# A weight ring of six buffers, a hand-over between two splitting engines, and q and k loads that wait for the gates

## The reference

```python
for t in range(S):
    m_new = np.maximum(f_gate[:, :, t] + m, i_gate[:, :, t])
    f_stab = np.exp(f_gate[:, :, t] + m - m_new)
    i_stab = np.exp(i_gate[:, :, t] - m_new)
    C = f_stab * C + i_stab * np.einsum('bhd,bhe->bhde', vt, kt)
    n = f_stab * n + i_stab * kt
    h_tilde = np.einsum('bhde,bhe->bhd', C, qt)
    denom = np.maximum(np.abs(np.einsum('bhd,bhd->bh', n, qt)), 1.0)
    y[:, :, t] = sigmoid(o_gate[:, :, t]) * h_tilde / denom
```

```python
x = (sigmoid(x @ w_gate) * (x @ w_val)) @ w_out            # layer 1
xn = x / np.sqrt(np.mean(x * x, -1) + 1e-6) * rms_g
x = (silu(xn @ w2_gate) * (xn @ w2_val)) @ w2_out          # layer 2
```

## Time and profile before

| what | value |
|---|---|
| median of 3 runs | 450.21 us (450.01 to 450.27) |
| the profiled execution | 450.15 us |
| its span, first to last instruction | 447.9 us |
| TensorE (PE) busy | 443.5 us, 99% |
| VectorE busy | 217.7 us, 49% |
| ScalarE busy | 183.6 us, 41% |
| GpSimd busy | 87.4 us, 20% |
| DMA traffic | 26.69 MB |

### The profile page before, as it was taken

One profiled execution on the slowest core, in us unless ns is written; L12 is line 12 of the kernel. 1 busy time (PEld: TensorE's weight loads), 2 busy tenths in 40 slices (PEclk: granted clock), 3 DMA queues, 4 the chain that ended last, 5 costly groups with the idle time before them and its releaser, 6 DMA issues.

```text
span 447.9 us, 10560 instructions
## 1 busy us (share of the span) xinstructions
PE 443.5 (99%) x4491; PEld 405.7 (91%) x4491; DVE 217.7 (49%) x475; ACT 183.6 (41%) x358; POOL 87.4 (20%) x131
## 2 busy tenths in 40 slices
PE   8999999999999999999999999999999999999997
PEld 5899999999999999988889988889988899888897
DVE  6879827854565456414432227560055730256510
ACT  7886277544753473214543154331033320133310
POOL 3569610112010200004656181000000000000000
PEclk9999999999999999999999999999999999999999
DMA  8975500321122114000433010000000000000000
GB/s 240 299 262 167 140 3 3 82 82 35 51 80 69 37 31 143 19 1 14 148 106 113 22 44 1 1 0 31 31 2 0 1 16 29 16 2 1 0 31 29
DMA packets 10430, 26.69 MB, mean 60 GB/s; under 512 B 1504, under 2 KB 4608, under 8 KB 10384
## 3 DMA queue, kind: packets, MB, share of 16 engines
q1 hardware_dynamic: 10128, 25.96, 19.1%
q10 hardware_dynamic: 256, 0.07, 0.1%
HBM read 23.97 MB, written 1.97 MB: 58 GB/s over the span
## 4 chain that ended last, share of the span: by engine, by line
PE 98%; DMA 1%; SPq 0%; ACT 0%; issue 0%
PE bank L1205 37%; PE bank L1156 21%; PE bank L1224 10%; PE bank L1226 9%; PE bank L1225 9%; PE bank L1063 3%; PE bank L1094 3%; PE bank L997 2%; PE bank L1082 1%; PE bank L1033 1%; PE bank L1103 1%; DMA step<-in_qk_t 1%; PE bank L1236 0%; PE bank L1249 0%; PE bank L1257 0%; PE bank L1047 0%
## 5 line engine op out<-in xcount | busy, mean ns | idle before, releaser
L1205 PE MATMUL bank<-x_hi,wgv_hi 64*128 64x512 f32 x576 | 106.0, 388 | 0.0
L676 ACT ACTIVATE sg<-bank 128x256 f32<-128x256 f32 (+1 forms) x96 | 47.1, 491 | 131.7 <-PE bank L1205 82.7
L1205 PE MATMUL bank<-x_lo,wgv_hi 64*128 64x512 f32 x480 | 94.0, 387 | 0.0
L947 DVE TENSOR_TENSOR bank<-sg,bank 128x256 f32<-128x256 f32 (+1 forms) x96 | 53.7, 560 | 55.8 <-ACT sg L676 54.1
L1156 PE MATMUL bank<-x_hi,wgv_hi 128*128 128x256 f32 x288 | 80.5, 291 | 0.0
L1156 PE MATMUL bank<-x_lo,wgv_hi 128*128 128x256 f32 x288 | 77.8, 283 | 0.0
L1224 PE MATMUL bank<-wo_hi,h_hi 128*128 128x320 f32 x240 | 75.5, 314 | 0.0
L1205 PE MATMUL bank<-x_hi,wgv_lo 64*128 64x512 f32 x384 | 75.2, 387 | 0.0
L1226 PE MATMUL bank<-wo_hi,h_lo 128*128 128x320 f32 x240 | 74.2, 309 | 0.0
L1225 PE MATMUL bank<-wo_lo,h_hi 128*128 128x320 f32 x240 | 74.2, 309 | 0.0
L945 DVE TENSOR_TENSOR sg<-sg,bank 128x512 f32<-128x512 f32 x36 | 24.8, 688 | 83.0 <-ACT sg L676 83.0
(11 more groups left out here) (143 smaller groups left out, 540.4 us busy)
## 6 DMA issues: line engine op xcount, KB each, us to landing
step<-in_qk_t SPq DMA_DIRECT2D x24, 192.0 KB, 3.8
step<-in_vok SPq DMA_DIRECT2D x12, 324.0 KB, 3.0
step<-in_w_gv SPq DMA_DIRECT2D x6, 576.0 KB, 3.7
raw_p<-in_w_gv SPq DMA_DIRECT2D x4, 576.0 KB, 5.2
raw_x<-in_w_gv SPq DMA_DIRECT2D x4, 576.0 KB, 6.7
step<-in_vok SPq DMA_DIRECT2D x10, 160.0 KB, 4.4
raw_p<-in_w_o SPq DMA_DIRECT2D x3, 480.0 KB, 3.2
y<-y_tok SPq DMA_DIRECT2D x9, 160.0 KB, 1.8
```

Source lines behind the costliest of these rows:

```text
L676: act.activation(sg_view(n), g_view(n), ACT.Sigmoid).then_inc(sg_done, 1)
L947: dve.tensor_tensor(v_view(n), sg_view(n), v_view(n), ALU.mult).then_inc(hf_done, 1)
L1205: mm = pe.matmul(ps(n), w, x, start=own and (s, p) == (0, 0), stop=last and not own)
```

## The change

Four edits:

1. SP waits for the gates' semaphore before it issues the loads of q and k, and with them every later load.
2. There are six raw buffers. Chunks 0 and 1 get one each of their own, and chunks 2 to 11 go round a ring of the other four. Chunks 4 and 5 no longer wait for a split; the load of chunk 4 is issued ahead of q and k of tile 3.
3. ScalarE waits for the splits of chunks 0 and 1 at tile 2, and for the last split at tile 5 in place of tile 4, because the buffers lie under other tiles now.
4. GpSimd waits for VectorE's split of chunk 7 before it starts on chunk 6.

```diff
-            under("pad0", [P, 4 * CW])
-            raw_x0 = under("raw_x0", [P, 4 * CW])
+            under("pad0", [P, 2 * CW])
+            raw_x0 = under("raw_x0", [P, 3 * CW])
+            raw_x2 = under("raw_x2", [P, 3 * CW])
...
-            under("pad1", [P, 4 * CW])
-            raw_x1 = under("raw_x1", [P, 4 * CW])
+            under("pad1", [P, 2 * CW])
+            raw_x1 = under("raw_x1", [P, 3 * CW])
+            raw_x3 = under("raw_x3", [P, 3 * CW])
...
-        raw0 = [raw_p[:, :], raw_x0[:, 0:3 * CW], raw_x1[:, 0:3 * CW], raw_q[:, :]]
+        raw0 = [t[:, :] for t in (raw_p, raw_q, raw_x2, raw_x3, raw_x0, raw_x1)]
+        RING = len(raw0) - B
+
+        def raw0_at(c):
+            return RING + c if c < B else (c - B) % RING
...
             def load_raw0(c):
-                if c >= len(raw0):
-                    wait_split(sp, c - len(raw0))
+                if c >= B + RING:
+                    wait_split(sp, c - RING)
                 src, w = raw_src(0, c)
-                s = c % len(raw0)
+                s = raw0_at(c)
...
             sp.dma_start(fi_r[:, :, :], gates[:, :, :]).then_inc(gates_in, 16)
+
+            sp.wait_ge(gates_in, 16)
             load_qk(0)
             load_qk(1)
...
             load_qk(2)
             load_vo(2)
+            load_raw0(4)
             load_qk(3)
             load_kn(2)
-            load_raw0(4)
             load_raw0(5)
...
                         for c in SPLIT_AT.get(slot, []):
+                            if c == BY_VECTOR[-1] - 1:
+
+                                wait_split(pool, c + 1)
                             split(0, c)
...
-                    act.wait_ge(raw0_in[c % len(raw0)], 16 * (c // len(raw0) + 1))
+                    act.wait_ge(raw0_in[raw0_at(c)], 16 * (1 if c < B else (c - B) // RING + 1))
...
-                    if n == 4:
+                    if n == B:
+                        for c in range(B):
+                            wait_split(act, c)
+                    if n == 5:
                         wait_split(act, WCH - 1)
```

More of the change, by code:

```diff
@@ L217, in raw_of @@
         def raw_of(lay, c):
-            r = raw1[c % len(raw1)] if lay else raw0[c % len(raw0)]
+            r = raw1[c % len(raw1)] if lay else raw0[raw0_at(c)]
             if c < GVC:
```

## The result

| | median | lowest to highest | executions |
|---|---|---|---|
| before | 450.21 us | 449.88 to 450.27 | 5 |
| changed | 457.31 us | 455.58 to 458.79 | 5 |

The ratio is 1.0164, with a 95% interval of 1.0134 to 1.0194. I had forecast 451.9 and a range of 450.6 to 454.0: the direction was right, the size and the range were wrong.

The account below looks back on a forecast made before the run. TensorE's own list was taken as the bound, with q and k what its start waits for. Edit 1's +2.0 less 0.3 gave +1.7 us, the other edits 0; on 450.15 this made 451.9 us, range 450.6 to 454.0.

Parts of the forecast that it names:

- What bounds the kernel: Whole kernel: TensorE's list bounds it, 98% of the chain; at the start TensorE waits for q and k until 5.61.
- Edit 1, when the scores start: Kernel start: gates' signal at 3.4, q and k landing 4.15 us after issue, first scores at 7.64 against 5.65.
- the predicted +1.7: Edit 1's net term at the start: +2.0 us delay less 0.3 from faster scores, with ends +0.6 and +2.5.
- The port rule: Gates' load: 16 partitions make it slow by itself, so the signal stays near 3.64, the term near +2.0.
- The step that failed: First scores: at the higher clock they take 1.04 and not 1.30 us, giving 0.26 us back.
- The low clock: First block: rival that TensorE works at 1.2 GHz after the longer pause; about 454 us, chance 0.14.
- the main case: Whole kernel: +1.7 us from the delayed start, other edits cost 0, giving 451.9 us; chance 0.62.
- The rival's price: First block at low clock: 1.2 to 2.7 us on top of the +2.0, for scores, eight 256-column decay matmuls and fillers.
- Edits 2 and 3: Raw buffers, load order and ScalarE's moved waits: nothing starts sooner or later on the chain, cost 0 each.
- Edit 4: Splits of chunks 6, 7, 11: chunk 7 takes 1.7 us; cover 1.0 us for chunk 6, 0.7 for 11; cost 0.
- The late hand-over: Slots needing chunk 6 or 11: rival that one misses its slot, 0.5 to 1 us more, 452.6 us; chance 0.08.
- the faster case: VectorE and GpSimd at 34.8 to 39.1: rival that ending their clash shortens the chain, at most to 449.2; chance 0.04.

Follow-up runs that it names:

- the eighth run: The changed kernel with 10 in place of 5 fillers in the first group: 451.40 us (451.17 to 451.54, 11 executions).
- the first run: The kernel before with one line added, SyncE's wait for the gates' signal before issuing q and k: 456.42 us (455.57 to 457.47, 4 executions).
- the second run: The changed kernel without SyncE's wait for the gates: 449.96 us; of ten executions eight took 449.77 to 450.04, two 456.23 and 456.50.
- the tenth: The changed kernel without SyncE's wait and with 7 in place of 5 fillers in the first group: 450.13 us (449.90 to 450.79, 12 executions).
- the eleventh: The kernel before with 7 in place of 5 fillers in the first group: 450.38 us (449.86 to 450.74, 12 executions).
- the seventh run: The kernel before with 6 first-group fillers and the gates' load issued by ScalarE: 450.96 us; four of 12 executions took 455.12 to 457.01.
- the ninth run: The changed kernel without the nine fillers between the numerators and the transposition of tile 1: 458.31 us (457.58 to 459.27, 4 executions).

## Why the prediction was wrong

**What bounds the kernel: right in the main, blind at one point.** The chain is TensorE's, and q and k were what the start waited for: with a steady clock their delay passes through to the end (1.35 us, the eighth run). But I took 450.2 for the kernel's one time. With nine fillers that end at 5.29 and scores at 5.65 its start sits at an edge where a third of its executions lose 6.3 us, and five executions didn't show it. The experiments move the number of fillers and the idleness together there, and don't tell which of the two makes the edge.

**Edit 1, when the scores start: right, mis-sized by 0.4 us.** The gates landed 2.4 us after their issue, what the interpolation had given, and I had taken more. The signal came at 3.1 and not 3.4. From the first issue to the landing it took 7.17 - 3.12 = 4.05 (predicted 4.15). So the scores started 1.56 us late and not 2.0. With a steady clock the net cost is 1.35 us (the eighth run), near the predicted +1.7 and inside its ends. So q and k did slow the gates, by 0.5 us in these two profiles (2.6 to 2.9 us in eight profiles with q and k issued behind on the same queue, 2.4 in five without). The port rule of the Trainium skill, "SBUF — State Buffer", section "Door 1: The DMA port swizzle", would have left the gates as late as before, and the measurement decides against that. Whether it explains why 96 KB take 2.4 and 8 KB 1.9 us no run tests.

**The step that failed: "If it has come to it by the time the delayed scores start, they take 1.04: 0.26 us back."** I counted the clock in the sum as a gain, put its loss there at nothing and left that to a rival with a chance of 0.14. The reason given, "that nine fillers have run as before", didn't hold: the same nine ran in the changed kernel and in the first run, with 2.19 and 1.97 us of idleness behind them, and all nine executions took over 455.5 us. In the changed kernel's profile the clock even had risen (its last filler took 0.38 and not 0.63 us from start to end), and the scores did take 1.26 us; then it fell at 8.1, and the work up to the first slot lost 5.7 us. The low clock was the main case.

**The rival's price was too low as well.** I had priced the low clock at 1.2 to 2.7 us above the delay; it cost 5.7. I charged it for two sets of scores, eight wide decay matmuls and the fillers. I had left out, without a reason, the narrow decay matmuls (+0.86 and +0.76) and the numerators (+1.44), which slow down nearly as the others do. These three make 3.06 of the 5.7. I had also taken the 1.30 us of before's first scores for the low pace and charged 0.26 for a set; the low pace is 1.92 to 1.99 us, and the second set lost 0.89. The fillers' share was about right: +1.16 against at most 1.5. The pieces of this one profile add up to its time, 450.15 + 1.56 + 5.7 = 457.4 against 457.31; that is a tally of what was measured and no second proof.

**Edits 2 and 3: right.** Cost 0 that can be told (the second run, and the tenth against the eleventh). The ring of six moved more than the loads of chunks 4 and 5. In the tenth run's profile against the eleventh's, chunk 4 is issued at 15.22 and not 19.63, q and k of tile 3 behind it at 15.69 and not 14.81, and GpSimd's wait of 4.5 us for values has gone. TensorE doesn't notice.

**Edit 4: right, with its numbers.** GpSimd and VectorE in the changed kernel:

```profile
42.01 0.55 DVE L924 TENSOR_TENSOR wgv_lo<-raw_q,wgv_hi 128x384 fp32r<-128x384 f32 x1
...
43.06 0.55 DVE L926 TENSOR_TENSOR wgv_hi<-raw_q,wgv_hi 64x384 fp32r<-64x384 f32 x1
...
43.69 2.00 POOL L486 TENSOR_TENSOR wgv_lo<-raw_p,wgv_hi 128x384 fp32r<-128x384 f32 x2 [2.02 <-DVE wgv_hi L926]
45.76 1.01 POOL L492 TENSOR_TENSOR wgv_hi<-raw_p,wgv_hi 64x384 fp32r<-64x384 f32 x1
...
56.13 3.07 POOL L502 TENSOR_TENSOR wo_lo<-raw_q,wo_hi 128x320 fp32r<-128x320 f32 x3
```

Chunk 7's split takes 42.01 to 43.61, 1.6 us and not 4.4. Chunk 6 is ready at 46.77 for a slot at 47.9, 1.1 us of cover (predicted 1.0). Chunk 11 is ready at 59.20 for 55.79 + 27 · 0.147 = 59.76, 0.6 us of cover (predicted 0.7). What VectorE gained was off the chain, as predicted. The late hand-over and the faster case didn't occur.

## What to carry to other kernels

A pause of TensorE can have a second price, apart from its length: if the clock is low behind it, the work that follows is slower by a factor of up to 1.9, here for 13.6 us. A pause lengthened from 0.36 to 2.2 us cost 1.4 us by itself and 5.7 through the clock. So price a delayed input twice, and look at what TensorE does while it waits. One to nine more fillers in the first group, which filled the wait or ended 0.5 to 0.7 us ahead of the input, cost at most some 0.6 us here and left none of 79 executions long as long as the gates' load stayed on SyncE. Where another load was moved beside them (the seventh run), four of 12 were long all the same. And when a kernel's start is near such an edge, a handful of executions doesn't show it: time it often enough to see whether its times fall into groups.

## What the runs showed of the hardware that was not expected

- TensorE had work without a pause and the clock stayed low. From 8.2 to 19.4 us it ran decay, score and numerator matmuls in the changed kernel at a granted clock of 0.50; the clock rose at 21.6, among the eight fillers.
- A pause behind a risen clock is not a loss by itself: 0.47 and 0.69 us of idleness (the eleventh and the eighth run) left the scores at 1.10 us, while behind 2.19 us the granted clock fell 0.8 us after the work had started again.
- The same program comes to the high clock in some executions and not in others (27 of 83 not). The Trainium skill, "TensorE: Matmul & The Clock Gate", part 1, says that the point of the switch varies from run to run with a monitor that doesn't start with the kernel; two groups of executions of one program agree with it, though no run shows why they fall apart. It also puts the cost of the ramp at under 1% of a typical kernel; here it is 6.3 of 450 us, 1.4%.
- The granted clock of a profile reads 1.00 until its first recorded fall. In the profiles of the second and the ninth run it reads 1.00 from 0 to 28 us, though scores take 1.99 and not 1.03 or 1.04 us. The pace of equal matmuls is the surer sign.
- A load of 96 KB was slowed by loads issued behind it: the gates took 2.4 us alone (five profiles), 2.6 to 2.9 with q and k issued behind on the same queue (eight profiles), and 4.4 when issued from ScalarE at the same time as them (one profile).
